# A chunked linear-attention layer: the bonus term as the diagonal of the scores, and all four array quarters used alike

## The chip, the cores and the metric

The kernel runs on one core of a Trainium2 chip. The metric is the device time of one execution in microseconds, median over runs.

## The reference

Three layers follow each other. Only the first is touched.

```
for t in range(S):                       # r, k, v, w: 4 batches, 8 heads, 768 tokens, 48 features
    y[t]  = r[t] @ (state + outer(u * k[t], v[t]))
    state = w[t][:, None] * state + outer(k[t], v[t])
h = x @ w_in; g = h * sigmoid(1.702 * h); x2 = g @ w_out          # 3072 tokens, 384 -> 2048 -> 384
# then soft experts: softmax over tokens gathers 32 slots, 8 experts on them, softmax over slots gives them back
```

The term with `u` is the bonus: for a token and a head it is the number sum_d(r*u*k) times the token's own v.

## The kernel before, in words

The tokens are cut into 24 chunks of 128 (6 per batch). For chunk n, VectorE (DVE) makes the running product of w (`decays`, L987), its inverse (`invert`, L1012), the decayed r (`decayed`, tile `rp`, L1021) and the grown k (`grown_keys`, tile `kd`, L1028). Features stand on partitions, even heads on 0 to 47 and odd heads on 64 to 111. TensorE turns kd (`turn_keys`, L1451), and ScalarE (ACT) copies it out as `kn` (L811).

TensorE works in slots F = 0 to 143 (and two more): a slot is `hidden_layer(F)` (nine products into `hps`, L1417), then the second matrix of slot F-2 (six or nine products into `acc`, L1552), then whatever tables hang on the slot: `part_at` (a part of a chunk's attention), `meeting_at` (a meeting) and the soft experts' gathers. Sixteen slots are a step; steps 0 to 2 have two chunks of tokens (256 columns), the others three. ACT makes in a slot `g` (L854) and `gh` (L865), DVE makes `gl` (L1185); `gl` of slot F is due at TensorE's second half of slot F+2. The engines' queues are in order, and each runs the same list of slots. At a step's start TensorE waits for the split tokens `xl` of the whole step (L544, DVE).

A meeting `meet(o, n)` holds the small products of two chunks: scores of chunk n (16, L1340), the products of chunk o's masked scores with v (`from_block`, 16, L1346), of its decayed r with the state (`from_state`, 16, L1352) and the sums of k and v of chunk n (`sum_tile`, 16, L1358; 8 for a batch's last chunk). Each product uses one quarter of the array: its input partitions are rows 0 to 63 or 64 to 127, its output partitions 0 to 63 or 64 to 127. Each is two matmul records in the trace. There are 22 meetings of a chunk n, 20 of them with an o; chunks 0 and 1 go through `output` at the start, and chunks 3 and 23 through `output` (L1311, L1317) in a slot of their own.

The bonus before: DVE multiplies r, u and k (`bonus`, tile `ruk`, L996; `products` L1003 for chunks 0 to 3), ACT and DVE split it in two (`rukh` L904, `rukl` L1212), TensorE sums over features with a matrix of ones (two products of 512 columns, L1570 and L1572, or `bonus_sums`, L1458, for chunks 0 to 3), DVE multiplies by v (`bonus_values`, L1053) and adds the meeting's output (`add_output`, L1091). Masked scores are score times a 0/1 mask (`mask_scores`, L1041), strictly above the diagonal.

The queue of SyncE (SP) loads in this order: raw r, k, v, w of chunk 0 and 1, six pieces of a test array, the first weights `stage`, `spare<-w_in`, raw of chunk 2, `spare<-w_out`, raw of chunk 3. `low_part(k)` (L1157, DVE) makes the low half of weight piece k, `high_part(k)` (L782, ACT) the high half.

## Time and profile before

| | |
|---|---|
| median of 3 runs | 597.43 us (597.21 to 599.02) |
| the profiled execution | 598.29 us, its span 596.6 us |
| busy: TensorE, DVE, ACT | 573.4, 329.6, 264.0 us |
| TensorE's granted clock | 0.992 of full speed |

A span runs from the first to the last instruction. A busy TensorE is not one at its peak, since matmuls overlap: the distance between starts tells what one costs.

### The profile page before, as it was taken

The numbers are of one execution on the slowest core, as the hardware profiler recorded it, in microseconds if no ns is written. First come the engines' busy times: TensorE is split into PE (matmuls) and PEld (weight loads), VectorE is DVE, ScalarE is ACT, GpSimd is POOL, SyncE is SP. The second block draws the span as 40 slices with busy tenths as digits, with TensorE's granted clock in tenths as the row PEclk, the third lists the DMA queues.
The fourth block names the chain that finished last, engine by engine and source line by source line (L and its number), as shares of the span: only waits on it lengthen the run. The fifth ranks groups of instructions, "written<-read, shape, count | busy, mean of one in ns | idle before, by whom it ended". The sixth has DMA issues, their size and how long they took to land.

```text
span 596.6 us, 15329 instructions
## 1 busy us (share of the span) xinstructions
PE 573.4 (96%) x6335; PEld 523.4 (88%) x6335; DVE 329.6 (55%) x713; ACT 264.0 (44%) x540; POOL 10.5 (2%) x28
## 2 busy tenths in 40 slices
PE   8889999999999999999999999999999999999983
PEld 6788989889989998999999999999999999998332
DVE  8778777657846664566445645576364224323304
ACT  3955444363463335333544344333533356554313
POOL 4010000000000000000000000000000000000000
PEclk9999999999999999999999999999999999999996
DMA  8994523323432322222212322232111197768728
GB/s 282 381 221 161 150 79 102 90 79 89 110 97 73 87 70 63 63 66 84 87 50 87 88 57 78 73 88 73 56 48 27 40 387 243 230 223 280 245 77 317
DMA packets 52983, 77.52 MB, mean 130 GB/s; under 512 B 4256, under 2 KB 33440, under 8 KB 52576
## 3 DMA queue, kind: packets, MB, share of 16 engines
q1 hardware_dynamic: 41872, 54.88, 28.8%
q10 hardware_dynamic: 10240, 18.50, 10.1%
q0 software_dynamic: 800, 3.15, 1.7%
q8 instruction: 51, 0.84, 0.6%
q14 instruction: 20, 0.16, 0.1%
HBM read 67.46 MB, written 9.04 MB: 128 GB/s over the span
## 4 chain that ended last, share of the span: by engine, by line
PE 83%; DMA 7%; DVE 3%; issue 3%; ACT 2%; SPq 2%; ACTq 0%; DVEq 0%
PE hps L1417 33%; PE acc L1552 32%; DMA spare<-w_in 4%; DMA w2s<-w 2%; PE zps L1340 2%; PE mps L1358 2%; PE yps L1352 1%; PE mps L1451 1%; PE mps L1635 1%; PE zps L1352 1%; PE mps L1668 1%; PE zps L1346 1%; DMA out<-obuf 1%; PE mps L1648 1%; PE hps L1712 1%
## 5 line engine op out<-in xcount | busy, mean ns | idle before, releaser
L1185 DVE TENSOR_TENSOR gl<-g,gh 128x384 fp32r<-128x384 f32 (+1 forms) x144 | 73.9, 513 | 209.0 <-ACT gh L865 208.9
L1417 PE MATMUL hps<-xh,wi_hi 128*128 128x384 f32 (+1 forms) x432 | 146.8, 340 | 3.5 <-ACT g L854 2.2
L1417 PE MATMUL hps<-xh,wi_lo 128*128 128x384 f32 (+1 forms) x432 | 137.2, 318 | 0.0
L1417 PE MATMUL hps<-xl,wi_hi 128*128 128x384 f32 (+1 forms) x432 | 137.0, 317 | 0.0
L854 ACT ACTIVATE g<-hps 128x384 f32<-128x384 f32 (+1 forms) x144 | 65.6, 455 | 146.4 <-PE hps L1417 146.2
L1552 PE MATMUL acc<-wo_hi,gl 128*128 128x384 f32 x384 | 129.2, 337 | 0.0
L1552 PE MATMUL acc<-wo_lo,gh 128*128 128x384 f32 x384 | 129.2, 336 | 0.0
L1552 PE MATMUL acc<-wo_hi,gh 128*128 128x384 f32 x384 | 129.0, 336 | 0.2 <-issue 0.2
L865 ACT ACTIVATE gh<-g 128x384 fp32r<-128x384 f32 (+1 forms) x144 | 70.5, 489 | 118.1 <-PE acc L1552 117.5
L1417 PEld LDWEIGHTS hps<-xh,wi_hi 128*128 128x128 f32 x432 | 81.2, 188 | 13.7 <-issue 5.3
L1417 PEld LDWEIGHTS hps<-xl,wi_hi 128*128 128x128 f32 x432 | 81.5, 189 | 0.9
L1417 PEld LDWEIGHTS hps<-xh,wi_lo 128*128 128x128 f32 x432 | 81.2, 188 | 0.0
L1552 PEld LDWEIGHTS acc<-wo_lo,gh 128*128 128x128 f32 x384 | 72.2, 188 | 0.3 <-issue 0.3
L1552 PEld LDWEIGHTS acc<-wo_hi,gh 128*128 128x128 f32 x384 | 72.2, 188 | 0.1
L1552 PEld LDWEIGHTS acc<-wo_hi,gl 128*128 128x128 f32 x384 | 72.1, 188 | 0.0
L1012 DVE TENSOR_TENSOR_SCAN inv<-raw,ends 112x516 f32<-112x516 f32 x24 | 29.6, 1233 | 0.8
L987 DVE TENSOR_TENSOR_SCAN decay<-raw,restart 112x516 f32<-112x516 f32 x24 | 29.4, 1224 | 0.6 <-DMA raw<-dmaj 0.6
L1358 PE MATMUL mps<-vn,kn 64*48 64x48 f32 x640 | 23.7, 205 | 1.1 <-issue 0.9
L996 DVE SCALAR_TENSOR_TENSOR ruk<-raw,ucols 112x128 f32<-112x128 f32 x80 | 23.2, 345 | 0.0
L1358 PEld LDWEIGHTS mps<-vn,kn 64*48 64x48 f32 x640 | 20.3, 121 | 1.4 <-issue 1.0
L1352 PE MATMUL zps<-rp,state 48*48 48x64 f32 x320 | 21.5, 216 | 0.0
L1352 PE MATMUL yps<-rp,midway 48*48 48x64 f32 x320 | 20.7, 216 | 0.0
(251 smaller groups left out, 734.2 us busy)
## 6 DMA issues: line engine op xcount, KB each, us to landing
w1s<-w SPq DMA_DIRECT2D x16, 768.0 KB, 6.6
w2s<-w SPq DMA_DIRECT2D x16, 768.0 KB, 6.2
raw<-dmaj ACTq DMA_DIRECT2D x40, 225.8 KB, 2.6
vn<-vnat SPq DMA_DIRECT2D x24, 192.0 KB, 2.5
tests<-wall SPq DMA_DIRECT2D x6, 768.0 KB, 15.0
out<-obuf SPq DMA_DIRECT2D x12, 384.0 KB, 4.0
raw<-dmaj ACTq DMA_DIRECT2D x20, 226.2 KB, 2.5
raw<-dmaj ACTq DMA_DIRECT2D x20, 225.3 KB, 2.5
```

Of the source, the lines that this page charges most:

```text
L854: act.activation(g32[F % 2][:, 0:wide], hps[F % 2][:, 0:wide], ACT.Gelu_apprx_sigmoid).then_inc(gelu_done, 1)
L865: act.activation(gh[F % 2][:, 0:wide], g32[F % 2][:, 0:wide], ACT.Copy).then_inc(gh_done, 1)
L987: dve.tensor_tensor_scan(flat[0], flat[1], flat[2], 1.0, ALU.mult, ALU.max).then_inc(scanned, 1)
L996: last = dve.scalar_tensor_tensor(ruk[n % 2][:, p, :], field(n, RR)[:, p], ucols[:, p:p + 1], field(n, KK)[:, p], ALU.mult, ALU.mult)
L1012: dve.tensor_tensor_scan(flat[0][:, ::-1], later, flat[1][:, ::-1], 1.0, ALU.mult, ALU.add).then_inc(inverted, 1)
L1185: dve.tensor_tensor(out=gl[F % 2][:, 0:wide], in0=g32[F % 2][:, 0:wide], in1=gh[F % 2][:, 0:wide].bitcast(fp32), op=ALU.subtract).then_inc ...
L1340: return pe.matmul(score_banks(n)[par][cols, p * HALF:(p + 1) * HALF], kd[n % 2][rows, p, cols], rp[n % 2][rows, p, cols], start=p == 0, s ...
L1346: return pe.matmul((zps, yps)[c][HALF * par:HALF * par + D, p * HALF:(p + 1) * HALF], vn[o % 2][rows, h * D:(h + 1) * D], scores[rows, par ...
L1352: return pe.matmul((zps, yps)[c][rows, p * HALF:(p + 1) * HALF], (state[o % 2], midway)[c][rows, p, :], rp[o % 2][rows, p, HALF * c:HALF * ...
L1358: return pe.matmul(sum_banks(n)[c][HALF * par:HALF * par + D, p * D:(p + 1) * D], kn[n % 2][rows, p, HALF * par:HALF * par + D], vn[n % 2] ...
L1417: last = pe.matmul(hps[F % 2][:, 0:wide], w[:, g, at:at + 128], v[i % 2][:, g, 0:wide], start=m == 0, stop=m == 3 * G - 1)
L1552: last = pe.matmul(acc[m][:, 0:DM], a[k][:, rows], w[:, f % CW, :], start=f == 0 and w is hi and a is gh, stop=f == NF - 1 and a is gl)
```

## The change

The array v is no longer loaded with features on partitions (field `VV`): the raw tile has three fields (NQ) in place of four. r and k are loaded a second time with tokens on partitions (`rknat`, tile `natural`), and u as a row for each partition (`u_row`). For chunks 2 to 23 `weigh` makes r*k, times u, and reduces over the features: one number for token and head (`bonus`). For chunks 0 and 1 TensorE makes it (`bonus_sums`, products with two columns). `mask_scores` fills the score tile with that number on the diagonal and zero elsewhere (`eye` times `bonus`), and copies the scores in above the diagonal with a predicated copy. The bonus then goes through `from_block`, and the output needs a copy alone (`take_output`, on ACT).

In the meeting, `from_state` used the two quarters with equal row and column half only. Now ACT copies half of rp, and half of state and midway, to the other partitions (`move_across`), and the two output halves with c != par read these copies, in the other two quarters. The order of the products is changed too, and chunks 3 and 23 now use `meet(o, None)`.

```diff
-        place_parts(2, scan=1, invert=1, grow=2, decayed=3, bonus_a=4, turn=4, bonus=6)
-        place_parts(3, scan=5, invert=7, grow=7, turn=8, decayed=8, bonus_a=8, bonus=10)
+        place_parts(2, scan=1, invert=1, grow=2, weigh=3, decayed=3, turn=4, mask=8, across=6)
+        place_parts(3, load_n=5, scan=5, invert=6, grow=6, decayed=7, turn=8, weigh=9, across=9)
...
-        low_at = {0: 2, 4: 3, 6: 4, 9: 5, 10: 6, 12: 7}
+        low_at = {0: 2, 4: 3, 9: 5, 10: 6, 12: 7}
+        low_behind = {5: 4}
...
                 if n < PRE:
-                    sp.wait_ge(uv_done, n + 1)
+                    sp.wait_ge(decayed_done, n + 1)
+                    sp.wait_ge(front, n + 1)
+                    sp.wait_ge(rk_made, n + 1)
                     load_raw(n + 2)
+                if n == 0:
+                    sp.dma_start(u_row[:, :], urow).then_inc(u_row_in, 16)
+                if n == 1:
+                    sp.dma_start(natural[:, :, :], rknat[PRE]).then_inc(rows_in, 16)
...
+            def move_across(n):
+                first, second = slice(0, D), slice(HALF, HALF + D)
+                if n > PRE:
+                    act.wait_ge(meetings, met_out[n - 1])
+                act.wait_ge(decayed_done, n + 1)
+                act.activation(rp_across[first], rp[n % 2][second, :, 0:HALF], ACT.Copy)
+                act.activation(rp_across[second], rp[n % 2][first, :, HALF:C], ACT.Copy)
+                act.wait_ge(state_done, n)
+                act.activation(across[first], state[n % 2][second], ACT.Copy)
+                act.wait_ge(midway_done, n + 1)
+                act.activation(across[second], midway[first], ACT.Copy).then_inc(moved_across, 1)
...
+            def weigh(n):
+                dve.wait_ge(rows_in, 16 * (n - PRE + 1))
+                done = 3 * (n - PRE)
+                dve.tensor_tensor(out=natural[:, 0], in0=natural[:, 0], in1=natural[:, 1], op=ALU.mult).then_inc(weighed, 1)
+                dve.wait_ge(u_row_in, 16)
+                dve.wait_ge(weighed, done + 1)
+                dve.tensor_tensor(out=natural[:, 0], in0=natural[:, 0], in1=u_row[:, :], op=ALU.mult).then_inc(weighed, 1)
+                dve.wait_ge(weighed, done + 2)
+                dve.tensor_reduce(bonus[n % 2][:, :], natural[:, 0].rearrange("t (h d) -> t h d", h=H), AX, ALU.add).then_inc(weighed, 1)
...
+                dve.tensor_tensor(out=scores[:, :, :, :], in0=eye[:, :].unsqueeze(1).unsqueeze(1).broadcast_to([C, 2, HP, HALF]),
+                                  in1=weight.unsqueeze(3).broadcast_to([C, 2, HP, HALF]), op=ALU.mult).then_inc(diagonal, 1)
...
+                    dve.wait_ge(y_done, n)
+                dve.wait_ge(diagonal, n + 1)
                 for par in range(2):
-                    dve.tensor_tensor(out=scores[:, par], in0=score_banks(n)[par].rearrange("s (p t) -> s p t", p=HP),
-                                      in1=mask[:, :].unsqueeze(1).broadcast_to([C, HP, HALF]),
-                                      op=ALU.mult).then_inc(scored, 1)
+                    dve.copy_predicated(scores[:, par], mask[:, :].bitcast(i32).unsqueeze(1).broadcast_to([C, HP, HALF]),
+                                        score_banks(n)[par].rearrange("s (p t) -> s p t", p=HP)).then_inc(scored, 1)
...
+                if n is not None:
                     for p in range(HP):
                         for c in range(2):
                             for par in range(2):
-                                last = from_block(c, par, p)
-                    last.then_inc(crossed, 1)
-                for p in range(HP):
-                    if o is not None:
-                        from_state(0, 0, p)
-                    last = sum_tile(0, 1, p, True)
-                    if o is not None:
-                        from_state(1, 1, p)
-                    if both:
-                        last = sum_tile(1, 0, p, True)
-                last.then_inc(half_summed, 1)
+                                score_tile(par, c, p)
+                    for p in range(HP):
+                        last = sum_tile(0, 1, p, True)
+                        if both:
+                            last = sum_tile(1, 0, p, True)
+                    last.then_inc(half_summed, 1)
                 if o is not None:
-                    pe.wait_ge(crossed, o + 1)
+                    for product in (from_block, from_state):
+                        for p in range(HP):
+                            for c in range(2):
+                                for par in range(2):
+                                    last = product(c, par, p)
+                if n is not None:
+                    pe.wait_ge(half_summed, n - PRE + 1)
                     for p in range(HP):
-                        for par in range(2):
-                            from_state(1 - par, par, p)
...
```

TensorE's queue, a meeting with both chunks, before the change; `rp_75`, `scores` and `vn_69` belong to chunk o, the other numbered tiles to chunk n, and each product's quarter follows from c and par in the code:

```order
L1340 MATMUL yps<-rp_76,kd_78 64x64
L1346 MATMUL zps<-scores,vn_69 48x64 x2
L1346 MATMUL yps<-scores,vn_69 48x64 x2
L1352 MATMUL zps<-rp_75,state_88 48x64
L1358 MATMUL mps<-vn_70,kn_84 48x48
L1352 MATMUL yps<-rp_75,midway 48x64
...
L1352 MATMUL yps<-rp_75,midway 48x64 [waits crossed]
L1352 MATMUL zps<-rp_75,state_88 48x64
...
L1358 MATMUL mps<-vn_70,kn_84 48x48 [waits half_summed]
L1358 MATMUL mps<-vn_70,kn_84 48x48 x3
```

The same meeting after the change, from the last score product on:

```order
L1348 MATMUL yps<-rp_76,kd_78 64x64
L1370 MATMUL mps<-vn_70,kn_80 48x48 x4
L1354 MATMUL zps<-scores,vn_69 48x64 x2
L1354 MATMUL yps<-scores,vn_69 48x64 x2
...
L1364 MATMUL zps<-rp_75,state_88 48x64
L1364 MATMUL zps<-rp_across,across 48x64
L1364 MATMUL yps<-rp_across,across 48x64
L1364 MATMUL yps<-rp_75,midway 48x64
...
L1370 MATMUL mps<-vn_70,kn_80 48x48 [waits half_summed]
L1370 MATMUL mps<-vn_70,kn_80 48x48 x3
```

The first half of the sums, which stood between products with the state, is now a block of its own ahead of `from_block`, and the second round of `from_state` behind a wait is gone.

DVE's queue in slots 13 and 14, ahead of the start of step 1, before (`decay_71` to `ruk_79` are chunk 4's, `xl_102` the last piece of tokens that slot 16 waits for):

```order
L1185 TENSOR_TENSOR gl_115<-g_1_110,gh_112 128x256 [waits mlp_done,gh_done]
L987 SCALAR_TENSOR_TENSOR decay_71<-raw_67,restart 112x516 [waits w_in0]
L996 SCALAR_TENSOR_TENSOR ruk_79<-raw_67,ucols 112x128 [waits k_in0,r_in0]
L996 SCALAR_TENSOR_TENSOR ruk_79<-raw_67,ucols 112x128
L1185 TENSOR_TENSOR gl_114<-g_0_109,gh_111 128x256 [waits mlp_done,gh_done]
L1008 RECIPROCAL ends<-decay_71 112x4 [waits scanned]
L1012 SCALAR_TENSOR_TENSOR inv<-raw_67,ends 112x516 [waits ends_made]
L544 TENSOR_TENSOR xl_102<-x,xh_101 128x3x128 [waits xh_done]
```

And after:

```order
L1207 TENSOR_TENSOR gl_115<-g_1_110,gh_112 128x256 [waits mlp_done,gh_done]
L1018 SCALAR_TENSOR_TENSOR decay_71<-raw_67,restart 112x516 [waits w_in0]
L1207 TENSOR_TENSOR gl_114<-g_0_109,gh_111 128x256 [waits mlp_done,gh_done]
L1038 RECIPROCAL ends<-decay_71 112x4 [waits scanned]
L1042 SCALAR_TENSOR_TENSOR inv<-raw_67,ends 112x516 [waits ends_made]
L1028 TENSOR_TENSOR natural<-natural 128x384 [waits rows_in]
L1031 TENSOR_TENSOR natural<-natural,u_row 128x384 [waits weighed,u_row_in]
L1033 TENSOR_REDUCE bonus_83<-natural 128x8 [waits weighed]
L544 TENSOR_TENSOR xl_106<-x,xh_105 128x3x128 [waits xh_done]
```

Two short products of `bonus` left the queue ahead of `xl`, and the three instructions of `weigh` came in.

DVE's queue in slots 3 and 4 after the change, where `natural` is needed for the first time (chunk 2); before, `rp` was followed by `gl`, one product and this same `wo_lo`:

```order
L1051 TENSOR_TENSOR rp_75<-raw_67,decay_71 112x512 [waits av_done,raw_in0]
L1028 TENSOR_TENSOR natural<-natural 128x384 [waits rows_in]
L1031 TENSOR_TENSOR natural<-natural,u_row 128x384 [waits weighed,u_row_in]
L1033 TENSOR_REDUCE bonus_83<-natural 128x8 [waits weighed]
L1207 TENSOR_TENSOR gl_114<-g_0_109,gh_111 128x256 [waits mlp_done,gh_done]
L1182 TENSOR_TENSOR wo_lo_60<-spare_125,wo_hi_59 128x1536 [waits hi_done]
```

`gl` of slot 4 and a weight's low half now stand behind a load that comes late in SP's queue.

## Rows read from the trace of the kernel before

**Rows 1.** The page: busy time and share of each engine.

```profile
PE 573.4 (96%) x6335; PEld 523.4 (88%) x6335; DVE 329.6 (55%) x713; ACT 264.0 (44%) x540; POOL 10.5 (2%) x28
```

**Rows 2.** TensorE's waits in the whole span: us in total, times, longest.

```profile
PE hps L1417 <- ACT g L854: 2.2, 1, 2.2
...
PE hps L1417 <- DVE xl L544: 1.0, 1, 1.0
```

**Rows 3.** Groups by form, TensorE: busy, mean ns, idle before.

```profile
L1570 PE MATMUL mps<-rukh,headsum 112*112 112x512 f32 x20 | 8.0, 399 | 0.0
```

**Rows 4.** The chain that ended last, in order of time, first 110 us.

```profile
10.97 21.34 DMA spare<-w_in
...
47.68 0.87 PE mps L1458 x8
...
61.98 0.88 PE mps L1458 x8
...
64.33 1.24 PE hps L1417 x9
...
92.52 0.24 PE mps L1570
92.76 0.23 PE mps L1572
```

**Rows 5.** Timeline of TensorE, one meeting: start, length, instruction.

```profile
216.07 0.27 PE L1340 MATMUL zps<-rp,kd 48*64 48x64 f32 x1
...
217.03 0.22 PE L1352 MATMUL zps<-rp,state 48*48 48x64 f32 x1
...
217.36 0.21 PE L1358 MATMUL mps<-vn,kn 64*48 64x48 f32 x2
...
217.43 0.22 PE L1352 MATMUL zps<-rp,state 48*48 48x64 f32 x1
...
217.93 0.54 PE L1358 MATMUL mps<-vn,kn 64*48 64x48 f32 x16
218.40 0.45 PE L1417 MATMUL hps<-xh,wi_hi 128*128 128x384 f32 x1
```

**Rows 6.** Timeline of TensorE, the end of the second `output` at the start.

```profile
21.73 0.25 PE L1317 MATMUL zps<-scores,vn 64*48 64x64 f32 x1
...
21.78 0.22 PE L1311 MATMUL zps<-rp,state 48*48 48x64 f32 x1
...
21.82 0.22 PE L1317 MATMUL zps<-scores,vn 64*48 64x64 f32 x1
```

**Rows 7.** Groups by form, DVE.

```profile
L996 DVE SCALAR_TENSOR_TENSOR ruk<-raw,ucols 112x128 f32<-112x128 f32 x80 | 23.2, 345 | 0.0
...
L1053 DVE TENSOR_TENSOR ybuf<-mps,raw 112x512 f32<-112x512 f32 x22 | 15.1, 685 | 0.0
...
L544 DVE TENSOR_TENSOR xl<-x,xh 128x384 fp32r<-128x384 f32 x22 | 11.9, 542 | 0.0
...
L1041 DVE TENSOR_TENSOR scores<-yps,mask 128x256 f32<-128x256 f32 x22 | 9.1, 413 | 0.0
```

**Rows 8.** Groups by form, ACT.

```profile
L865 ACT ACTIVATE gh<-g 128x256 fp32r<-128x256 f32 x48 | 20.0, 418 | 25.9 <-PE acc L1552 25.5
```

**Rows 9.** Timeline of DVE, slots 3 and 4.

```profile
40.80 0.69 DVE L1021 TENSOR_TENSOR rp<-raw,decay 112x512 f32<-112x512 f32 x1
...
43.29 1.75 DVE L1157 TENSOR_TENSOR wo_lo<-spare,wo_hi 128x1536 fp32r<-128x1536 f32 x1
```

**Rows 10.** Timeline of SP's DMA queue, the last load of the start.

```profile
25.70 0.53 SPq L692 DMA_DIRECT2D phis<-phi  x1
```

**Rows 11.** DMA issues: KB each, median us from issue to landing.

```profile
phis<-phi SPq DMA_DIRECT2D x1, 48.0 KB, 17.9
```

**Rows 12.** Timeline of DVE, slots 12 to 14.

```profile
69.26 0.43 DVE L1185 TENSOR_TENSOR gl<-g,gh 128x256 fp32r<-128x256 f32 x1 [1.16 <-ACT gh L865]
...
75.42 0.53 DVE L544 TENSOR_TENSOR xl<-x,xh 128x384 fp32r<-128x384 f32 x1
```

More of the change, by code:

```diff
@@ L44 @@
 WP = 4
-W, RR, KK, VV = range(4)
+W, RR, KK = range(3)
 SMALLEST = 1e-30
@@ L52 @@
 ON_ACT, ON_DVE = (0, 1, 2, 4), (3, 5)
+NQ = 3
 GEN_DMAS = 16 * 2 * (1 + HP)
@@ L57, with attention_mlp_soft_experts @@
 INSIDE = float(128 * len(ON_DVE) * (TW // SPAN)) * (HIGH - LOW)
-def attention_mlp_soft_experts(nc, dmaj, vnat, wall, ucol, w_in, w_out, phi, w1, w2, scratch, out):
+def attention_mlp_soft_experts(nc, dmaj, vnat, rknat, wall, ucol, urow, w_in, w_out, phi, w1, w2, scratch, out):
     fp32 = mybir.dt.float32
@@ L99, in attention_mlp_soft_experts @@
         attn_at = place[0]
-        raw = [sb(f"raw{i}", [R, 4, HP, C + 1]) for i in range(2)]
+        raw = [sb(f"raw{i}", [R, NQ, HP, C + 1]) for i in range(2)]
         vn = [sb(f"vn{i}", [C, DM]) for i in range(2)]
@@ L106, in attention_mlp_soft_experts @@
         kd = [sb(f"kd{i}", [R, HP, C]) for i in range(2)]
-        ruk = [sb(f"ruk{i}", [R, HP, C]) for i in range(2)]
-        rukh = sb("rukh", [R, HP, C], f32r)
-        rukl = sb("rukl", [R, HP, C], f32r)
         kn = [sb(f"kn{i}", [C, HP, R]) for i in range(2)]
+        natural = sb("natural", [C, 2, DM])
+        u_row = sb("u_row", [C, DM])
+        bonus = [sb(f"bonus{i}", [C, H]) for i in range(2)]
         scores = sb("scores", [C, 2, HP, HALF])
@@ L126, in attention_mlp_soft_experts @@
         above = [sb(f"above{i}", [128, TW], f32r, at=step_at + i * TW * 4) for i in range(2)]
+        rk = [sb(f"rk{i}", [R, HP, C], at=step_at + i * HP * C * 4) for i in range(2)]
         x = sb("x", [128, G, ST])
@@ L215, in attention_mlp_soft_experts @@
         raw_in = [sem(f"raw_in{i}") for i in range(2)]
-        field_in = [[sem(f"{name}_in{i}") for i in range(2)] for name in ("w", "r", "k", "v")]
+        field_in = [[sem(f"{name}_in{i}") for i in range(2)] for name in ("w", "r", "k")]
         vn_in = [sem(f"vn_in{i}") for i in range(2)]
@@ L1032, in mask_scores @@
                 if n < PRE:
-                    dve.wait_ge(z_done, n + 1)
+                    dve.wait_ge(bonus_made, n + 1)
                 else:
-                    dve.wait_ge(meetings, met_in[n])
+                    dve.wait_ge(weighed, 3 * (n - PRE + 1))
+                weight = (acc[1][:, 0:H] if n < PRE else bonus[n % 2][:, :]).rearrange("t (p r) -> t r p", r=2)
                 if n and n <= PRE:
@@ L1114, in start_up @@
                     dve.tensor_copy(fold[rows], ident[rows, rows])
+                for c in range(2):
+                    rows = slice(HALF * c, HALF * (c + 1))
+                    last = dve.tensor_copy(eye[rows], ident[rows, rows])
+                last.then_inc(eye_made, 1)
+                decays(1)
+                dve.wait_ge(eye_made, 1)
                 mask_scores(0)
-                decays(1)
                 first_state(0)
@@ L1217, in _ @@
                     before, n = meeting_at[F]
-                    if before is not None:
-                        add_output(before)
                     if n is not None:
@@ L1347, in from_block @@
                                      vn[o % 2][rows, h * D:(h + 1) * D], scores[rows, par, p, :],
[L1348 removed]
+                                     start=n is None and p == 0, stop=False, skip_group_check=True)
                 def from_state(c, par, p):
[L1351 to L1353 removed]
+                    out, rows = slice(HALF * par, HALF * par + D), slice(HALF * c, HALF * c + D)
+                    if c == par:
+                        held, asked = (state[o % 2], midway)[c], rp[o % 2][rows, p, HALF * c:HALF * (c + 1)]
+                    else:
+                        held, asked = across, rp_across[rows, p, :]
+                    return pe.matmul((zps, yps)[c][out, p * HALF:(p + 1) * HALF], held[rows, p, :], asked,
+                                     start=False, stop=True, skip_group_check=True)
                 def sum_tile(c, par, p, first):
@@ L1454, in bonus_sums @@
             def bonus_sums(n):
-                pe.wait_ge(ruk_made, n + 1)
+                pe.wait_ge(rk_made, n + 1)
+                pe.wait_ge(diagonal, n)
                 for p in range(HP):
-                    last = pe.matmul(bonus_bank(n)[0:R, p * C:(p + 1) * C], heads_u[p][:, :], ruk[n % 2][:, p, :],
-                                     start=True, stop=True)
-                last.then_inc(u_done, 1)
+                    last = pe.matmul(acc[1][:, 2 * p:2 * p + 2], rk[n][:, p, :], heads_u[:, p, :], start=True, stop=True)
+                last.then_inc(bonus_made, 1)
             def state_sums(n):
```

218 lines of the change are left out of this document (84 added, 134 removed).

## Prediction

> **What bounds the kernel now.** The page first: TensorE is busy 573.4 of 596.6 us, DVE 329.6 and ACT 264.0 [rows 1]. A busy TensorE isn't yet the bound, so TensorE's waits come next. In the whole span it waits for another engine only in single places of 2.2 us and less: once for `g` at the start and once for `xl` ahead of slot 16 [rows 2]. The chain that ended last says the same: the head of the program hangs on a load (`spare<-w_in`, issued at 10.97, landed 21.34 later, at 32.3), and behind it nearly every step is TensorE's own work, the bonus products among it [rows 4]. So between slot 2 and the tail, what is taken out of TensorE's queue comes off the time one for one, unless another engine's work gets in its place. DVE and ACT count only where TensorE already waited, or where they lose more than their slack.
>
> **The large term: the bonus leaves TensorE.** From chunk 4 on two products of 512 columns go, for each of 20 chunks [rows 3]. Their records are 0.4 us long, but matmuls overlap: in the chain they take 0.24 and 0.23 us [rows 4], and that is their price. 20 x 0.47 = 9.4 us. Below it can't well be: they stand between full-array products and the chain gives the distance between starts. For chunks 2 and 3 four exact fp32 products go, 0.87 and 0.88 us in the chain [rows 4], 1.75 together. No product takes their place: the diagonal rides in the score tiles that are multiplied with v anyway.
>
> **Chunks 3 and 23** had 12 products a quarter in use (two rounds of `from_state` in two quarters, one of `from_block` in four). The one in the chain starts at 61.98 + 0.88 = 62.86 and ends at 64.33 [rows 4], 1.47 us. One round of three goes, so a third of all but the edges: 0.45 each.
>
> **The meeting.** One with both chunks goes from 216.07 to 218.40, 2.33 us, in four parts [rows 5]: scores and `from_block` to 217.03 (0.96), one round of `from_state` with half the sums beside it to 217.43 (0.40), the second round, in the same two quarters, to 217.93 (0.50), the other half of the sums and the switch to the full array to 218.40 (0.47). The change takes out the second round, 0.50. But it puts the first half of the sums in a block of its own, in the two quarters that `from_state` did not use before, and it hides behind nothing there unless the other two quarters run ahead into `from_block`. Its eight records a quarter start from 217.03 to 217.36, so 0.047 each, 0.37 in all. How far can a quarter run ahead of products that stand earlier in the queue? Two places bound it. In the mixed part the last sum starts at 217.36, the `from_state` record of the same round at 217.43, and it stood in front: a lead of 0.07 us that grew round by round with no stop. At the end of a start `output` two `from_block` records start at 21.73, before a `from_state` record that is earlier in the queue starts at 21.78 and before the first `from_block` product of all, 21.82 [rows 6]; a lead of 0.09. So products of different quarters do pass each other, by about one product as far as any row shows. With no lead the meeting is 0.96 + 0.37 + 0.42 + 0.47 = 2.22, with full independence 1.85, with the lead seen (0.07) 2.15. I take the last, nearest to the rows: 0.18 saved, bounds 0.11 and 0.48, 20 meetings.
>
> The Trainium skill (TensorE: Matmul & The Clock Gate, Part 3, Packing small matmuls) says matmuls start and end strictly in program order and that only weight loads are pulled ahead. By that rule the new block of sums is paid in full and the meeting saves the 0.11 alone; that is a rival below. The two leads of 0.07 and 0.09 us speak against its letter, though not for a long lead.
>
> **The start.** Chunks 0 and 1 are 903 KB each of raw (112 x 2064 x 4 bytes); a quarter of each goes ahead of `spare<-w_in` in the same queue, 452 KB. The queue's last load is issued at 25.70 [rows 10] and lands 17.9 later [rows 11], at 43.6. Between 32.3 and 43.6 it moved raw of chunks 2 and 3, two vn of 192 KB, `spare<-w_out` of 768 and the last 48, 3006 KB, so 266 KB a us. 452 KB are 1.7 us. TensorE waits 2.2 us at that place [rows 2], for ACT that splits this weight first. I take 1.1, since ACT's own list before it is nearly as long; bounds 0 and 1.7.
>
> **New waits before slot 16.** These eat a part. (a) `natural` of chunk 2 lands late: after `spare<-w_in` (31.2 now) come raw 677, u_row 192, vn 192, weight 768, raw 677 and itself 384, 2890 KB or 10.9 us, so 42.1. DVE is through `rp` at 41.4 [rows 9], 1.1 earlier now, 40.3, and stands 1.8 us; then `weigh`: two products of 128 x 384, 0.54 each as `xl` [rows 7], and a reduce of the same size, which no row shows and I put at the same 0.54, 1.65 together. Behind it are `gl` of slot 4 and the low half of a weight, which started at 43.29 [rows 9] and now at about 44.1, where 42.2 would be in step. That lateness of 1.9 is worked off by what DVE drops in slots 4 to 10 (three products of 0.68 [rows 7], the adds, now ACT's copies); against it weigh of chunk 3 comes in slot 9, ahead of a weight's low half and of the masks that slot 10 waits for. I put 0.9 on the waits in slots 8 and 10, bounds 0 and 1.9. (b) Ahead of slot 16 DVE is busy without a break from 69.26 to the end of `xl`, 75.95 [rows 12], and TensorE waits 1.0 for it [rows 2]. There `weigh` comes in (1.65) and half a `bonus` goes (two of 0.345, less overlap, 0.5 [rows 7]): 1.15 more. The start of this stretch hangs on TensorE's slot 12, early by 1.1 + 1.75 + 0.45 + 0.18 - 0.9 = 2.6. So slot 16 starts 2.6 - 1.15 = 1.45 earlier than before. That is all the first 76 us give.
>
> **After slot 16** DVE per chunk drops four of 0.345, two of 0.69 and two adds, and gains 1.65, a diagonal of 512 elements (0.68 as L1053 [rows 7]) and two predicated copies in place of two products of 0.41 [rows 7]. It gets less to do. ACT gains six copies of at most 0.42 [rows 8] and drops one split, some 1.9 us a chunk, 42 in all on 264 busy of 597: hidden in its waits. They stand behind the meeting or a slot later, and what queues behind them, the next `g`, waits for TensorE's next first half (1.6 us) anyway. `rp_across` is due three slots later. The added 159 KB of load per chunk meets idle queues. Nothing here costs.
>
> **The sum.** 1.45 (to slot 16) + 9.4 + 19 x 0.18 = 3.4 + 0.45 (chunk 23) = 14.7 us. The profiled execution took 598.3, so 583.6; the median of 3 was 597.4, 0.9 lower, so 582.7. I say 583.
>
> **Rivals.**
> (1) Strict order of matmuls: each meeting saves 0.11, so 19 x 0.07 = 1.3 less gain, 584. For it: nothing shows a lead of over one product. Against it: [rows 5, 6].
> (2) Quarters are independent as far as the queue reaches: the sums vanish behind `from_block`, 0.48 a meeting, 19 x 0.30 = 5.7 more gain, 577.3; without the early waits too (2.05), 575.3. For it: the lead in the mixed part grew without a stop.
> (3) The start gives nothing: `spare<-w_in` lands as before or ACT is the limit (1.1), and the late `natural` costs its 1.9 in full (1.0 more): 585 to 586.5 with strict order.
> (4) Slower than before: the predicated copy reads PSUM and a mask and may be far slower than the product it replaces. `gl` of the slot after a meeting then comes late. DVE's other work after the meeting is 1.65 + 0.35; `gl` is due two full slots and a first half later, some 8.5 us after the meeting's end. To lose 14.7 us over 20 meetings each must stall 0.75, so the pair of copies must last over 6.5 us, 3 us and more for one, eight times the 0.41 of the product. Same time as before: just under that. The nearest rows give no sign.
>
> **How the numbers follow.** Forecast 0.52 (own range 581 to 585), strict order 0.15, independent quarters 0.15, a poor start 0.10, slower 0.05, no change 0.03. Cases 1 to 3 all are faster by over 0.3% (1.8 us, about what this kernel's measurement can tell): 0.92, 0.03, 0.05. The range takes rival 2 to 576 and rival 3 to 588, the latter with 1.5 for a predicated copy of twice the time where DVE is tight before slot 16.
>
> **What would show it.** Right: no records of 512-column bonus products; first half of slot 16 at about 74.5; meetings of 2.15 us; TensorE's waits few. The meeting decides rivals 1 and 2: in its timeline, whether the first `from_block` record in quarters (0,0) and (1,1) starts with the last sums or with the first. A wait of DVE for the load of `natural` of some 1.8 us shows (a). I am wrong if TensorE's waits name the masks, `across` or `gl` in steps 3 to 8, or if the head of the chain stays where it was.

## The result: 591.12 us against 597.43

The changed kernel takes 591.12 us (median of 7, 590.05 to 594.51), the kernel before 597.43 (7 runs, 596.27 to 599.02): a ratio of 0.9902, 95% interval 0.9881 to 0.9923. It is faster, by under half of what was forecast, and outside the range. The profiled execution took 590.05 us, the fastest of the seven; its span is 588.1. Each ratio here and below is against runs of the kernel before taken beside it (their medians: 597.43 us here, 597.42, 596.73 and 596.57 below), so it differs a little from the ratio of two medians.

The page of the changed kernel, where [rows 1] stand before:

```profile
PE 561.5 (95%) x6279; PEld 513.7 (87%) x6279; DVE 316.3 (54%) x632; ACT 301.1 (51%) x650; POOL 10.5 (2%) x28
```

TensorE's waits, us in total, times, longest, as in [rows 2]:

```profile
PE hps L1422 <- DVE xl L544: 4.4, 3, 2.4
PE hps L1422 <- ACT g L888: 1.6, 1, 1.6
...
PE yps L1319 <- DVE grown L1098: 1.4, 1, 1.4
...
PE zps L1310 <- issue: 1.0, 1, 1.0
```

TensorE lost 11.9 us of busy time, and the span 8.5. The wait for `xl` is there three times and not once. What the waits do not show is the clock. The windows of the start (TensorE's busy time and instructions, granted clock, DMA share, GB/s), of the changed kernel:

```profile
16.00:19.00 3.00, 2.07 (x53) 0.97 1.03 415
19.00:22.00 3.00, 2.97 (x34) 0.50 1.00 409
22.00:25.00 3.00, 3.00 (x46) 0.50 1.04 378
25.00:28.00 3.00, 2.65 (x50) 0.89 1.10 311
```

For 6.8 us, from 18.8 to 25.7, TensorE runs at 1.2 instead of 2.4 GHz. In the trace of before the clock is 1.00 in all these windows.

Where the time went is read from the start of each slot's first half in the timeline, lead of the changed kernel over the one before:

```
                       before    after    lead     forecast for the stretch, measured
slot 0                  30.14    33.61   -3.47
slot 6                  45.33    48.36   -3.03     to slot 6:      +1.1    -3.0
slot 12                 66.44    67.53   -1.09     6 to 12:        +1.5    +1.9
slot 16                 76.01    78.56   -2.55     12 to 16:       -1.15   -1.5
slot 31                120.45   120.94   -0.49
slot 32                123.79   125.03   -1.24
slot 47                167.61   168.08   -0.47
slot 48                170.95   172.54   -1.59
slot 143               537.74   530.27   +7.47     16 to 143:     +13.25  +10.0
end of the span        596.6    588.1    +8.5      tail:            0      +1.0
```

The steady part is nearly as forecast: from slot 48 to 143 the lead grows by 9.06 us, where the forecast's terms for these slots (14 bonuses, 14 meetings, chunk 23) add up to 9.55. What is missing between 16 and 143 is missing before slot 48. The slots that held the bonus products are 0.43 to 0.47 us shorter (slot 58: 3.68 before, 3.25 now). Slot 59 with a meeting takes 5.42 us where it took 5.58, 0.16 less, 0.18 forecast. The timeline of that meeting, against [rows 5]:

```profile
215.92 0.27 PE L1348 MATMUL zps<-rp,kd 48*64 48x64 f32 x1
...
216.44 0.39 PE L1370 MATMUL mps<-vn,kn 64*48 64x48 f32 x10
216.64 0.25 PE L1354 MATMUL zps<-scores,vn 64*48 64x64 f32 x1
216.66 0.26 PE L1370 MATMUL mps<-vn,kn 64*48 64x48 f32 x4
...
217.66 0.52 PE L1370 MATMUL mps<-vn,kn 64*48 64x48 f32 x14
218.11 0.45 PE L1422 MATMUL hps<-xh,wi_hi 128*128 128x384 f32 x1
```

From 215.92 to 218.11 are 2.19 us, where it was 2.33. The sums stand alone in their two quarters from 216.44 to 216.64, and products of the other quarters start (216.64) while the last sums, which are ahead of them in the queue, still do (216.66).

New operations by form, DVE and ACT (busy, mean ns, idle before), beside [rows 7, 8]:

```profile
L1033 DVE TENSOR_REDUCE bonus<-natural 128x8 f32<-128x384 f32 x22 | 12.2, 553 | 0.8
L1080 DVE COPY_PREDICATED scores<-mask,zps 128x256 f32<-128x256 int32 x22 | 9.9, 451 | 2.9
```
```profile
L827 ACT ACTIVATE rp_across<-rp 48x256 f32<-48x256 f32 x22 | 9.2, 417 | 0.6
L832 ACT ACTIVATE across<-midway 48x192 f32<-48x192 f32 x22 | 8.0, 363 | 0.3
```

The predicated copy takes 0.45 us where the product took 0.41 (rival 4 needed 3 us). So rival 4 is out.

### The profile page after: what moved, and what is told of

The parts are those of the page before. It is cut to its first block, busy times and chain, and to the rows that moved or that the text cites. A ratio compares the mean times of both kernels' runs of the same rounds, so it can differ in the third digit from the quotient of the medians.

```text
span 588.1 us, 15153 instructions
## 1 busy us (share of the span) xinstructions
PE 561.5 (95%) x6279; PEld 513.7 (87%) x6279; DVE 316.3 (54%) x632; ACT 301.1 (51%) x650; POOL 10.5 (2%) x28
## 4 chain that ended last, share of the span: by engine, by line
PE 86%; DVE 5%; ACT 3%; issue 3%; DMA 2%; SPq 0%; DVEq 0%; ACTq 0%
PE hps L1422 33%; PE acc L1557 32%; PE mps L1370 2%; PE zps L1348 2%; PE mps L1456 2%; PE acc L1671 1%; DMA raw<-dmaj 1%; PE mps L1625 1%; DMA out<-obuf 1%; PE mps L1638 1%; PE zps L1354 1%; PE mps L1702 1%; PE mps L1658 1%; PE hps L1702 1%; PE zps L1364 1%
## 5 line engine op out<-in xcount | busy, mean ns | idle before, releaser
L843 ACT ACTIVATE ybuf<-zps 112x256 f32<-112x256 f32 x22 | 8.5, 386 | 34.2 <-PE mps L1370 33.3
L1354 PE MATMUL zps<-scores,vn 64*48 64x64 f32 x352 | 16.9, 219 | 0.8 <-issue 0.8
L1348 PEld LDWEIGHTS zps<-rp,kd 48*64 48x64 f32 x352 | 12.1, 134 | 6.3 <-issue 6.3
```

Of the source, the lines that this page charges most:

```text
L1348: return pe.matmul(score_banks(n)[par][cols, p * HALF:(p + 1) * HALF], kd[n % 2][rows, p, cols], rp[n % 2][rows, p, cols], start=p == 0, s ...
L1354: return pe.matmul((zps, yps)[c][HALF * par:HALF * par + D, p * HALF:(p + 1) * HALF], vn[o % 2][rows, h * D:(h + 1) * D], scores[rows, par ...
```

## The experiments

**The start and its filler.** TensorE's queue in `start_up` holds filler products (`keep_warm`), which write a bank that nobody reads. One run adds filler to the changed kernel, the other takes filler from the kernel before.

```diff
 state_sums(0)
-keep_warm(WARM)
+keep_warm(WARM + WARM + WARM)
 outputs(0)
-keep_warm(WARM)
+keep_warm(WARM + WARM)
...
 bonus_sums(1)
+keep_warm(WARM)
 pe.wait_ge(y_done, 1)
```

> The changed kernel with more filler matmuls of 128 x 256 at the start (six more ahead of the first output, three more ahead of the second chunk's scores, three behind its bonus sums). Theory A: the start lost 3.5 us because TensorE, left with two-column bonus products and a longer wait, was granted half its clock from 18.8 to 25.7 us. Then the clock stays 1.00 over the start, slot 0 starts near 30.2 instead of 33.6, and the time falls by 2.5 to 4 us against the changed kernel (591.1), to 587.5 or so. Rival B: DVE's longer chain at the start (diagonal and predicated copies) is what delays it; then the clock is repaired but slot 0 still starts at 32 or later, and the time falls by under 1 us.

Measured: 591.46 us (589.77 to 591.91, 4 runs), ratio 0.9878 (0.9847 to 0.9908). That is no gain that these executions can tell, and yet the trace shows one in the start: half clock from 20.4 to 23.8 only, and slot 15 is 0.50 us ahead of before, where the changed kernel is 1.08 behind. In the trace it is lost in the next slots: behind the wait for `xl` (2.45 us, ending at 76.98) the clock falls for 3.4 us. The products of slot 17, whose distance is 0.12 us at full clock, start 0.22 apart:

```profile
81.06 0.41 PE L1422 MATMUL hps<-xh,wi_lo 128*128 128x256 f32 x1
81.28 0.41 PE L1422 MATMUL hps<-xh,wi_hi 128*128 128x256 f32 x1
```

From slot 18 on the two kernels' slots start within 0.02 us of each other. That they come out level is chance: slot 16 had started 1.58 us earlier, and slots 16 and 17 took 1.56 more.

In the changed kernel's own trace the same wait of 2.44 us was followed by no fall. That trace is the exception: five traces here have this wait of 2.44 to 2.46 us ahead of slot 16, and in the other four (this one, and those of the meeting's order, the bonus alone and the copies' place below) the clock falls behind it, and slots 16 and 17 take 6.2 to 6.3 us together where the changed kernel's take 4.7. In the eight traces with a wait of 0.7 to 1.2 us there it does not fall. The changed kernel's other executions have mean clocks of 0.981 to 0.985 where the profiled one has 0.989, so most of them probably pay this 1.5 us too; no trace shows it. The clock is not all of it, either: one execution of this run took 591.32 us with a mean clock of 0.991.

This trace's tail is 1.6 us longer than the changed kernel's. The clock falls in it, at 573.3, but it does so at 575.8 and 572.5 in the traces of the next two changes, whose tails are no longer than the changed kernel's. From the second on its stores take 4.7 to 5.6 us to land, where they take 2.9 to 4.0 in the changed kernel; the clock is not shown to cost anything there.

> The kernel before with its three groups of filler matmuls between the first chunk's bonus sums and the second chunk's scores taken out; nothing else differs. Theory A: the clock falls to half somewhere between 12 and 26 us, slot 0 starts 2 to 4 us later than 30.1, and the time rises by 2 to 4 us over 597.4. Rival B (the clock's fall in the changed kernel is a by-product that costs little): the time stays within 1 us of 597.4 even where the clock falls.

The diff takes out the three filler groups around `state_sums(0)` and `outputs(0)` of the kernel before. Measured: 598.22 us (595.88 to 600.19, 10 runs), ratio 1.0004 (0.9985 to 1.0023). Its trace has half clock from 14.8 to 21.6, slot 3 starts 2.25 us later than in before, and 2.09 of it are still there in slot 143. But that trace is the slowest of ten executions, which scatter over 4.3 us, and the interval ends at 1.4 us more than before: the rise of 2 to 4 us that was expected is refuted, and rival B, within 1 us, is what came. One trace shows that the start of before can lose its clock without filler; in the median that costs less than this run can tell.

**`xl` ahead of `weigh`.** On DVE in each step's slot 14, of the changed kernel:

```profile
76.25 0.53 DVE L1028 TENSOR_TENSOR natural<-natural 128x384 f32<-128x384 f32 x1
76.89 0.56 DVE L1031 TENSOR_TENSOR natural<-natural,u_row 128x384 f32<-128x384 f32 x1
77.48 0.55 DVE L1033 TENSOR_REDUCE bonus<-natural 128x8 f32<-128x384 f32 x1
77.95 0.55 DVE L544 TENSOR_TENSOR xl<-x,xh 128x384 fp32r<-128x384 f32 x1
```

The same four stand from 122.71 and from 170.22 on, ahead of slots 32 and 48.

```diff
-if (F, "weigh") in part_at:
+if (F, "weigh") in part_at and F % NF != 14:
     weigh(part_at[F, "weigh"])
...
     rest_x(dve, *split_now(F))
+if (F, "weigh") in part_at and F % NF == 14:
+    weigh(part_at[F, "weigh"])
```

> The changed kernel with the three instructions of weigh placed behind the split tokens xl in slot 14 of a step. Theory A: TensorE's waits for xl at the starts of steps 1, 2 and 3 (2.4, 0.95 and 1.0 us) go or fall to what the kernel before had (1.0 once), so the time falls by 2.5 to 3.5 us, to about 588. Rival B: xl is late because ACT's gh and xh are late; then the waits stay and the time falls by under 1 us.

Measured: 588.89 us (587.26 to 592.03, 4 runs), ratio 0.9833 (0.9804 to 0.9862). TensorE waits 0.7 us once for `xl`, where it waited 4.4 in three. From slot 15 to 143 the trace gains 11.0 us on before, the changed kernel's 8.6: 2.4 of the 3.7 us come back, since slots 16, 32 and 48 grow, by 0.55, 0.66 and 0.2. This profiled execution started 5.0 us late (half clock from 12.6 to 26.3); that of the run below has the same start.

**The meeting's order.** The sums of the first half share the array with `from_block` of the two other quarters, round by round, as do the last sums with `from_state`; the middle has four quarters each round.

```diff
 for p in range(HP):
     last = sum_tile(0, 1, p, True)
+    if o is not None:
+        from_block(0, 0, p)
     if both:
         last = sum_tile(1, 0, p, True)
+    if o is not None:
+        from_block(1, 1, p)
 last.then_inc(half_summed, 1)
...
+if o is not None and n is not None:
+    for p in range(HP):
+        from_block(0, 1, p)
+        from_state(0, 0, p)
+        from_block(1, 0, p)
+        last = from_state(1, 1, p)
...
 for p in range(HP):
+    if o is not None:
+        from_state(0, 1, p)
     last = sum_tile(0, 0, p, not both)
+    if o is not None:
+        last = from_state(1, 0, p)
     if both:
         last = sum_tile(1, 1, p, False)
```

> The changed kernel with the products of a meeting in another order: every off-diagonal quarter's product is queued beside one of a diagonal quarter (first sums beside from_block, the other from_block beside from_state, the other from_state beside the last sums), so that no quarter stands idle for a block. Theory A (a quarter runs ahead of earlier products by about one product only, so the block of sums is paid in the changed kernel): a meeting takes 1.85 instead of 2.17 us, 20 x 0.3, and the time falls by about 6 us, to 585. Rival B (what limits a meeting is something the quarters share, issue or a bank, and not the order): the meeting stays at 2.1 or more, the time within 1.5 us of 591.

Measured: 588.06 us (586.92 to 588.44, 4 runs), ratio 0.9822 (0.9795 to 0.9849), 3 us under the changed kernel, although its trace starts 5.0 us late too. The meeting goes from 217.88 to 219.76 in the timeline:

```profile
217.88 0.27 PE L1348 MATMUL zps<-rp,kd 48*64 48x64 f32 x1
...
218.39 0.22 PE L1354 MATMUL zps<-scores,vn 64*48 64x64 f32 x1
...
219.76 0.44 PE L1436 MATMUL hps<-xh,wi_hi 128*128 128x384 f32 x1
```

1.88 us, where the changed kernel takes 2.19; slot 59 takes 5.11 where it took 5.42. That is 0.45 less than the 2.33 of before, nearly the 0.48 that rival 2 put on independent quarters, and it is got by another order of the same products. The quarters were not independent over the block of eight sums; as neighbours in a round of four the products come within 0.03 us of the 1.85 that the prediction worked out for full independence.

**The two halves of the change apart, and the copies' place.** First the bonus on the diagonal alone: `from_state`, the order of the meeting and the condition before it as in before, and no `move_across`.

```diff
...
-    out, rows = slice(HALF * par, HALF * par + D), slice(HALF * c, HALF * c + D)
-    if c == par:
-        held, asked = (state[o % 2], midway)[c], rp[o % 2][rows, p, HALF * c:HALF * (c + 1)]
-    else:
-        held, asked = across, rp_across[rows, p, :]
...
+    rows = slice(HALF * par, HALF * par + D)
+    return pe.matmul((zps, yps)[c][rows, p * HALF:(p + 1) * HALF], (state[o % 2], midway)[c][rows, p, :],
+                     rp[o % 2][rows, p, HALF * c:HALF * (c + 1)], ...)
...
-if (F, "across") in part_at:
-    move_across(part_at[F, "across"])
```

> The change's bonus part alone: bonus as the diagonal of the scores, the products of the meeting in the order and shape of before, no copies across partitions. Forecast from the sum as corrected: the changed kernel's 591.1, plus 0.16 for each of 20 meetings (3.2), less the 1.3 that its copies on ScalarE cost the x2t copies in slots 20 to 41: 593.0, between 592 and 594.5; each bonus slot still 0.46 us shorter than in before. Rival (the copies across partitions cost more than the meetings gain): not above 591.1.

Measured: 592.59 us (591.94 to 592.87, 4 runs), ratio 0.9932 (0.9908 to 0.9955). Slot 58, which had a bonus before, takes 3.22 us instead of 3.68, slot 59 with its meeting 5.56 instead of 5.58. So the bonus on the diagonal gives some 0.7% of the 1.0% gained, and the copies across partitions with the new order 0.3%, with intervals that overlap.

```diff
-if (F, "across") in part_at:
-    move_across(part_at[F, "across"])
...
 act.activation(x2t[:, :, m * C:(m + 1) * C], ...).then_inc(x2t_done, 1)
+if (F, "across") in part_at and late:
+    move_across(part_at[F, "across"])
```

(`late`: the slots that turn the tokens of the soft experts; in all others `move_across` stays where it was, behind the split of x.)

> The changed kernel with move_across behind the x2t copy in the slots that turn the tokens of steps 1 and 2, nothing else. If the copy across partitions is what makes TensorE wait for x2t there, slots 37 and 41 lose their 0.5 us and slots 20 to 24 some 0.6, so 590.0 to 590.5 against 591.1. Rival: those slots are long because the copies of kn stand ahead of x2t, or because a wait moves to the next slot: 591.1, the sum of slots 36 to 38 unchanged at 7.65 us.

Measured: 589.79 us (589.30 to 589.92, 4 runs), ratio 0.9880 (0.9857 to 0.9903). By the time alone that is not clearly more than the changed kernel's gain, for the intervals overlap. The trace shows it slot by slot: 37 and 41 take 2.50 us each, as before, where the changed kernel takes 3.00; slots 20 and 24 lose 0.35 and 0.22, and no slot beside them grows, 1.6 us together. The timelines of ACT, changed kernel first: `x2t` behind the last of four copies, and ahead of the first.

```profile
140.39 0.36 ACT L832 ACTIVATE across<-midway 48x192 f32<-48x192 f32 x1
140.78 0.49 ACT L953 ACTIVATE x2t<-mps 128x384 f32<-128x384 f32 x1
```
```profile
140.08 0.49 ACT L954 ACTIVATE x2t<-mps 128x384 f32<-128x384 f32 x1
140.59 0.42 ACT L827 ACTIVATE rp_across<-rp 48x256 f32<-48x256 f32 x1
```

**All repairs together.** Filler (54 products of 256 columns in the start instead of 30), `xl`, the meeting's order and the copies' place, each edited as above; and the filler with `xl` alone. The filler is longer than in the first run:

```diff
-keep_warm(WARM)
+keep_warm(4 * WARM)
 outputs(0)
-keep_warm(WARM)
+keep_warm(3 * WARM)
...
 bonus_sums(1)
+keep_warm(WARM)
 pe.wait_ge(y_done, 1)
 state_sums(1)
+keep_warm(2 * WARM)
 pe.wait_ge(scored, 4)
```

> All repairs at once on the changed kernel: more filler products in the start, xl ahead of weigh in each step's slot 14, the meeting's products mixed over the array's quarters, and move_across behind the x2t copy. Theory of start, clock and xl (what was forecast and not given lies in the half-clock stretch of the start, in the waits for xl and what the clock does behind them, and in the x2t copies): from the changed kernel's 591.1 us it takes 2.5 for the start, 2.2 for xl, 1.0 for x2t and 3.0 for the quarters, and about 1 more because no fall of the clock follows an xl wait: 581.5, between 580 and 584, with slot 16 starting no later than 78.5 us in the trace and every slot of the late steps more than 12 us ahead of before. Rival (the start's loss is taken up by a later wait whatever is done to it): the gains of the two earlier runs alone, 591.1 less 2.2 less 3.0, 586.

> The changed kernel with more filler products in the start and with xl ahead of weigh in slot 14, nothing else. Theory: the filler alone gave nothing because the wait for xl in slot 15 let the clock fall again and took back what the start had won; with xl early the start's gain stays, so this is 2 to 3 us under the version with xl alone (588.9): 586.5, clock above 0.988, and slot 16 at most 0.5 us later than in before. Rival: the start's gain goes to another wait behind slot 14 (weights still landing): 588.9, as with xl alone.

Measured: all together 581.29 us (578.58 to 581.78, 5 runs), ratio 0.9727 (0.9701 to 0.9753); filler and `xl` 586.80 (584.92 to 588.87, 4 runs), ratio 0.9822 (0.9794 to 0.9851). Both times are those of the theory, and the first has slot 16 at 77.71 and slot 143 with a lead of 15.96 us. But that filler and `xl` gain more than `xl` alone (0.9822 against 0.9833) is not shown, and the trace does not support the reasons: the clock in the start is 1.00, slot 9 is 0.3 us ahead of before, and slot 16 is 1.98 behind, not 0.5. TensorE stops for 2.35 us in the middle of a meeting's sums, in slot 9, with no engine waited for and no product missing, and the clock falls behind it (0.50 from 61.5 to 64.9). The stop is in the trace of all together too, 1.9 us.

```profile
61.02 0.29 PE L1372 MATMUL mps<-vn,kn 64*48 64x48 f32 x3 [2.35 <-issue]
```

**Is the stop instructions on their way?** The next runs write each filler group as 512 and 256 columns (36 products instead of 54, so with their weight loads 36 instructions fewer), repeat all together beside it, and undo the filler alone.

```diff
-WARM = (256, 256, 256)
+WARM = (512, 256)
```

> The version with all repairs, with each filler group written as one product of 512 columns and one of 256 instead of three of 256: 36 filler products in place of 54, as many columns as the start needs, and so 36 fewer instructions ahead of slot 8. In the two traces with the longer filler TensorE stands 1.9 and 2.4 us in the meeting of slot 8 with nothing to wait for, where the changed kernel stands 0.8. If that stand is its instructions arriving late and more filler instructions make it longer, it is back at 0.8 us or less, slot 9 starts under 6.2 us after slot 8, and the time is 1 to 2 us lower: 580.0 against 581.3. Rival: the stand has nothing to do with the number of instructions: it stays near 2 us and the time at 581.3.

> The version with all repairs once more, beside the two others on the same chip: 581.3, 580.0 to 582.5, with a stand of TensorE of 1.9 to 2.4 us in slot 8.

> All repairs but the one of the start: xl early, the meeting mixed over the quarters, move_across behind x2t, and the filler of the changed kernel. If the start's half-clock stretch costs what the traces show, this is 3 us slower than with the longer filler: 584.5 (583.5 to 586), with a mean clock below 0.986. Rival (the start's loss is taken up by later waits): 581.3, the same as with it.

(Where these say slot 8 and slot 9, the slots are 9 and 10: they were counted one too low. The 0.8 us at which the first says the changed kernel stands is not this stop either: it is in slot 10, ahead of chunk 3's `from_block`, and the traces of the wide filler and the old start name the masked scores as what ends it, 0.82 and 0.84.) Measured: wide filler 579.53 us (578.07 to 579.88, 5 runs), ratio 0.9700 (0.9677 to 0.9723); all again 581.14 (578.64 to 581.65, 5 runs), ratio 0.9723 (0.9696 to 0.9750); old start 581.70 (578.94 to 582.76, 5 runs), ratio 0.9738 (0.9711 to 0.9766). The timeline of all again, and its DMA queue of instructions in the microsecond in which the stop begins (57 to 58: packets, MB, share):

```profile
57.63 0.22 PE L1369 MATMUL zps<-rp_across,across 48*48 48x64 f32 x1
60.02 0.21 PE L1369 MATMUL yps<-rp_across,across 48*48 48x64 f32 x1 [2.18 <-issue]
```
```profile
q8 instruction: 1, 0.02, 8.5%
```

With the wide filler slot 10 starts 4.97 us behind slot 9, where the repeat has 6.95, with no stop in the meeting; the time is 1.6 us lower, with intervals that overlap. So the stop hangs on how many instructions stand ahead of it. The Trainium skill (Advanced Engine Details and Errata, ISA Cache) says that instructions are held in lines of 16 KB, 256 instructions each. The packet of 0.02 MB agrees with that size, but it is no evidence of a late block: a packet like it moves between 57 and 60 us in the traces without a stop too, at 57.6 with the wide filler.

The traces have better evidence. Count TensorE's instructions (weight loads, matmuls and its semaphore instructions) from the start of the trace to each stop of over 0.3 us that names no engine. (Left out are stops at a product for which other traces name the engine: the first of slot 2, the first `output`, and chunk 3's `from_block`.)

```
instructions  TensorE stops for                                      where
ahead
  449         0.48 us in before, 0.45 to 1.12 in the changed kernel  sums of chunk 1, 18.6 to 19.5 us
              and four others
  705         0.35 to 0.65 us in the three traces of the long filler filler, 23.6 to 24.1 us
 1504         1.9, 2.35, 2.2 us in the same three                    slot 9; sums in one, from_state in two
 2784         0.90 us in before, 0.97 with before's filler out       sums of slot 26
```

705 is 449 and 256; 2784 is 1504 and five times 256; between 705 and 1504 the program branches around a part that isn't executed. The number stays while the product changes, and so does it between kernels with different fillers. So TensorE stops at the border of a block of 256 of its instructions, and the arrival of the next block is the reading left. What filler changes is where a border falls. The small products of slot 9's meeting are 256 instructions and pass in 2 us. The long filler puts the border six instructions before the meeting's end, right behind this rush; the wide one puts it behind the meeting, in slot 10, where TensorE waits 0.82 us for the masked scores anyway. The kernel before has such a stop as well:

```profile
110.11 0.56 PE L1358 MATMUL mps<-vn,kn 64*48 64x48 f32 x15 [0.90 <-issue]
```

No trace of a changed kernel has it: slot 26 is 1.24 us shorter in the changed kernel, where slots 35, 39 and 43, with the same kind of work, are 0.1 shorter. So about 1.1 us of the 10.0 between slots 16 and 143 are no term of the forecast, but luck with a border.

The run with the old start falls out of the theory: 584.5 expected, 581.7 measured, 0.6 over the runs with the longer filler and not 3. Its five executions suggest why, time and mean clock: 578.94 and 0.995, 579.28 and 0.988, 581.70 and 0.984, 581.88 and 0.981, 582.76 and 0.978. The old start does not always cost. The profiled one is the first, and its start stays at full clock:

```profile
16.00:19.00 3.00, 2.29 (x53) 2.08 (x53) 2.10 (x5) 1.54 (x2) 0.00 (x0) 1.00 1.03 415
19.00:22.00 3.00, 2.55 (x46) 2.34 (x48) 1.85 (x5) 2.97 (x4) 0.00 (x0) 1.00 1.00 412
```

(the last three columns are clock, DMA share and GB/s). Against the wide filler, which brings no stop, the old start is 2.2 us slower in the median; against the long one 0.6, and the long one has its stop of some 2 us in each of its three traces. The intervals of all three ratios overlap, so the times alone show no price of the start. I had taken the long filler as free.

The traces show one. Six kernels have the changed kernel's start word for word; their profiled executions differ in how long the clock is halved before slot 6, and slot 6 starts the later the longer:

```
                     half clock, us    slot 6 behind before, us
old start                  0                 0.83
bonus alone                3.4               1.63
copies' place              6.8               2.75
changed kernel             6.8               3.03
meeting's order           13.7               4.52
xl ahead of weigh         17.1               6.26
```

## Why the prediction was wrong

**The step that failed is "The start"**, +1.1 forecast and -3.0 measured, 4.1 of the 6.2 us between forecast and trace. It priced a load that lands earlier and looked at nothing else in these 30 us. `spare<-w_in` did land at 31.6, 0.7 earlier than [rows 4], but nobody waited for it: ACT reaches it only at 33.37, held up by TensorE and DVE. The step left out that TensorE has less to do there. Its bonus products now have two columns, and it has nothing left to do at 11.51, where that came at 12.02; and `grown`, behind the diagonal and the masked copy of chunk 0 on DVE, comes 0.3 us later. So TensorE idles 1.39 us where it idled 0.57, before and after:

```profile
12.13 0.36 DVE L1071 TENSOR_TENSOR grown<-yps,midway 112x192 f32<-112x192 f32 x1
12.59 0.23 PE L1311 MATMUL yps<-rp,midway 48*48 48x64 f32 x1 [0.57 <-DVE midway L1065]
```
```profile
12.44 0.36 DVE L1098 TENSOR_TENSOR grown<-yps,midway 112x192 f32<-112x192 f32 x1
12.89 0.22 PE L1319 MATMUL yps<-rp,midway 48*48 48x64 f32 x1 [1.39 <-DVE grown L1098]
```

At 19.03 it has idled 0.96, where it idled 0.48; this is the stop after 449 instructions, and not DVE's doing. During it the clock falls. What that costs is told by the table of starts: with 6.8 us of half clock slot 6 is 3.03 us behind before, with none 0.83. So 2.2 are the clock's, and the other 1.9 against the forecast are the idle time and the load that gains nothing. Of seven executions of the changed kernel the mean clock is 0.981 to 0.989, of before in the paired runs 0.989 to 0.994, and the profiled execution is the fastest of the seven; so halved clock, in the start or behind the wait for `xl`, costs the median rather more than it costs the trace.

**"After slot 16 nothing here costs" failed for the rest**: 13.25 forecast, 10.0 measured, and without the lucky border of slot 26 some 8.9. The step weighed DVE's total work and saw it fall. But the row of work that ends in `xl` grew, and this is what TensorE waits for at the start of slots 32 and 48 too: 0.75 and 1.12 lost. It was priced for slot 16 alone (1.15, measured 1.5, and 1.5 more in the traces where the clock falls behind it), one step short of asking where else the same list of work recurs. And ACT's copies were "hidden in its waits" by their sum; in slots 20, 24, 37 and 41 they stand ahead of `x2t`, for which TensorE waits at once, 1.6 us together by the trace of the run that moved them.

**Right:** the bonus products at 0.47 (0.46), the meeting at 0.18 (0.16) by the lead of about one product, chunk 23 at 0.45 (0.44), the predicated copy near its product. With the strict order that the Trainium skill (TensorE: Matmul & The Clock Gate, Part 3) states for matmuls a meeting would save the 0.11 of rival 1; 0.16 lies between that and the forecast, and in the timeline above a product of another quarter starts 0.02 us ahead of sums that stand before it. As a guide to what to write the rule holds better than I gave it credit for: quarters fill only with products that are neighbours in the queue, and putting them there gained 0.31 a meeting more.

**Right by luck:** slots 6 to 12, forecast at 1.5, gave 1.9. Of the parts, slot 10 should have been 1.3 us shorter without its bonus and with a round less for chunk 3, and is as long as before (4.95), for TensorE now waits there for a weight's low half and for the masked scores. In its place slots 7 and 8 are 1.3 us shorter, since waits of before for `wi_lo` and `kd` are gone, which nothing had forecast. And the load of `natural` landed when the prediction said (42.3, forecast 42.1), but DVE, late by the start, reached it only at 44.39 and did not wait; the 1.8 us of sign (a) are not in the trace.

Not foreseen: the tail, 1.0 us shorter from slot 143 to the end in the trace, 0.7 of it behind the last copies to `obuf`. The last five of the twelve stores take 4.5 to 4.9 us to land in the trace of before, 3.9 to 4.0 in the changed kernel's, and up to 5.6 in that of the longer filler, so it is hardly the change's doing; the cause is open.

**Left open:** why the clock falls in some executions and not in others behind the same idle times (1.39 and 0.96 us in the changed kernel's start and in the old start run; 2.44 us ahead of slot 16, without a fall in one trace of five). And why the next block of instructions comes late at some borders and in time at others.

## What to carry to other kernels

Before a change to the head of a kernel is priced by a load, list what TensorE does there microsecond by microsecond, with its granted clock: an idle time that grows from 0.6 to 1.4 us, with another that grows from 0.5 to 1.0, can cost 2 more behind it, in some executions. Work that leaves an engine's queue can be what makes it idle. When work is added ahead of something that an engine waits for, look up every place where the same list recurs, and the place in the queue rather than the sum. Products that use different quarters of the array have to be neighbours in the queue; and filler is not free, for it moves the borders of the blocks of 256 instructions, and one of them may land behind a rush of small products. The version with all of this, at 579.5 us, is 3.0% faster than before, three times the gain of the change as made.

## What the hardware showed unasked

The clock's fall behind a wait: 2.4 us of idle time ahead of slot 16 cost 1.5 us more in the next two slots in four traces, and nothing in a fifth. Stops of TensorE of 0.35 to 2.35 us mostly amid small products, 32 records of which pass in 0.7 us, that wait for no engine; they come after 449, 705, 1504 and 2784 of its instructions, whole multiples of 256 apart within each pair. A predicated copy of 128 x 256 out of PSUM takes 0.45 us, 0.04 more than a product; a copy of 48 x 256 across partitions on ACT takes 0.42.
